# Attention scores in groups of 64 keys, q's decay from two small tables, and x's operands made in the order of use

## Chip, cores and metric

The kernel runs on one core of one Trainium2 chip. The metric is the device time of one execution in microseconds. Five engines work side by side on their own instruction streams: TensorE (PE; its weight loads are shown as PEld), VectorE (DVE), ScalarE (ACT), GpSimd (POOL) and SyncE (SP), which here issues nearly all DMAs. They meet at semaphores alone.

## The reference

Three stages follow each other. What the first computes is what the change mostly touches:

```python
gamma = 1.0 - 2.0 ** (-5.0 - np.arange(H, dtype=np.float32))
scale = 1.0 / np.sqrt(D)
state = np.zeros((B, H, D, D), dtype=np.float32)
for t in range(S):
    state = gamma[None, :, None, None] * state + np.einsum('bhd,bhe->bhde', k[:, :, t], v[:, :, t])
    y[:, :, t] = scale * np.einsum('bhd,bhde->bhe', q[:, :, t], state)
...
h = x @ w_in                                   # 3072 x 512 by 512 x 2048
g = np.where(h > 0.0, h, alpha * (np.exp(np.minimum(h, 0.0)) - 1.0))
x = g @ w_out                                  # back to 512
...
h = x @ w_in2                                  # 512 x 1024
solu = h * softmax(h); ln = layernorm(solu) * g_ln
out = ln @ w_out2
```

B = 4 sequences, H = 8 heads, S = 768 positions, D = 64. All inputs are float32.

## The kernel before

**Attention.** A sequence is cut into six chunks of C = 128 positions. A step s (there are NS = 12) takes the same chunk of two sequences. Inside a chunk the work is: `scores(s)`, K times Q for each of 8 heads and both sequences (16 matmuls of 64 rows, 128 keys by 128 queries); `key_values(s)`, the chunk's own K times V, for the state (16 matmuls, 128 rows by 64 by 64); `values(s)`, V times the masked scores A (16 matmuls); and `carried(s)`, the state from the chunk before times Q (16 matmuls of 64 by 64 by 128). Scores lie in PSUM with the key on the partition and the query on the free axis. DVE multiplies them by `causal`, a table of ones and zeros (`apply_mask`, line 877), so an entry whose query is before its key is computed and thrown away. Each float32 matmul appears in the trace as two weight loads and two matmul records, so that a group of 16 is "x32". PE goes through a step in the order scores, key_values, values, carried; in the first chunk of a pair of sequences (s = 0 and 6) there is no carried, and in the last (s = 5 and 11) it is scores, carried, values.

The decays are put into the operands: q is multiplied by gamma^(t+1)/8 (`decay_q`: DVE for s < EARLY = 2, POOL after that), v by its inverse (`decay_v`: ACT, and POOL for half of the heads at s < 2), and the state by gamma^128 (`decay_state`, POOL, line 492). q's table `q_decay` is 128 x 512. It is made on the chip: two rows `q_rows` are spread over 128 partitions by one float32 matmul (line 756) that stands between two series of warming matmuls on zeros (`WARM = (8, 4)`), DVE takes it from PSUM for step 0, and ACT copies it to SBUF for the others (line 1236).

**Loads.** Per step SP loads q, k, v and kn (k in its natural layout), 512 KB each, into one of three slots; step s + 3 is asked for when PE has ended step s (`load_step`, line 348). For s of 2 and more the order is q, v, k, kn. POOL's program in attention is, step by step: decay_q(s + 1), decay_state(s), at s = 6 and 7 two sums each for the first weights (`sum_u`), and from s = 9 on three `split_u_lo` each.

**The first MLP.** Both products are done to float32 precision from split operands (hi and lo parts, three matmuls for one), and the first by a Strassen-Winograd scheme with seven products M1 to M7 for each pair of features tiles n: `up_pair(n)`, which works in the order M1, M6, M2, M7, M5, M4, M3. Each product is six 128 x 128 x 512 matmuls (lines 656 to 658). Its right operands are seven tiles of x, called B11, B21, T1, T3, T2, B22, T4; their hi parts are made by ACT (line 1229) and their lo parts by DVE (`split_x_lo`, line 909) in the order of the list `MADE`. M1 needs B11, M6 needs T2, M2 needs B21, M7 needs T3, M5 needs T1, M4 needs T4, M3 needs B22. For the first block of 512 x-columns three lo parts are made inside the attention loop (s = 8, 9, 10) and four after it. `keep_u2(0)`, which adds M1 to M6 and on which M7 waits, stands on DVE behind these four.

Of the kernel before, what the change touches and what calls it, by code (L numbers as in the profile page):

```python
# [28 lines left out]
ND = 2 * NF1  # L29
WARM = (8, 4)  # L30
EARLY = 2
# [19 lines left out]

def build(nc, units, w1, w_in2, w_out2, g_ln, tables, q_table, x_dram, x2_dram, out):
    f32, f32r = mybir.dt.float32, mybir.dt.float32r
# [3 lines left out]
    with ctx:  # L57
# [72 lines left out]
        def two_chunks(name, at):  # L130
# [7 lines left out]
             for s in range(2)]  # L138
        decays = place("decays", C + 2 * H, f32, E_AT + 2 * K2)
        causal, v_decay, state_decay = decays[:, 0:C], decays[:, C:C + H], decays[:, C + H:C + 2 * H]  # L140

        y_at = [GH_AT, GH_AT + 4096, GH_AT + 8192, WLO_AT + 2 * K2, WLO_AT + 4 * K2, WLO_AT + 6 * K2,
# [5 lines left out]
        q_decay = place("q_decay", HH * C, f32, U3_AT)  # L148

        q_rows = place("q_rows", HH * C + P, f32, XL_AT)  # L150
        warm = place("warm", 512, mybir.dt.bfloat16, XH_AT)
# [15 lines left out]
        ps = ctx.enter_context(nc.psum_tensor("ps", [P, 8 * 512], f32))[:, :].rearrange("p (b c) -> p b c", c=512)  # L167

        def ps_scores(one, h):
            return ps[:, 2 * one + h // HH, (h % HH) * C:(h % HH + 1) * C]  # L170

# [46 lines left out]
        v_in = [sem(f"v_in{s}") for s in range(SLOTS)]  # L218
        q_rows_in = sem("q_rows_in")
        q_decay_spread = sem("q_decay_spread")  # L220
        q_decay_kept = sem("q_decay_kept")
        decays_in = sem("decays_in")
# [86 lines left out]

        MADE = [B11, B21, T1, T3, T2, B22, T4]  # L310
        SUMS = [T1, T3, T2, T4]
# [159 lines left out]
        def _(pool):  # L471
# [45 lines left out]
            for s in range(EARLY):  # L517
                decay_v(s)
            pool.wait_ge(q_decay_kept, 1)
            for s in range(NS):  # L520
# [59 lines left out]
        def _(pe):  # L580

            def scores(s):
                slot = s % SLOTS
                pe.wait_ge(k_in[slot], 16 * loads(s))
                for one in range(2):
                    if s < EARLY:
                        pe.wait_ge(q_early, 2 * s + one + 1)
                    else:
                        pe.wait_ge(q_decayed, 2 * (s - EARLY) + one + 1)
                    if s > 0:  # L590

                        pe.wait_ge(masked, 2 * s - 1 + one)
                    q, k = q_sb[slot][:, one, :], k_sb[slot][:, one, :]
                    for hh in range(HH):
                        for h in (hh, HH + hh):
                            c = slice(hh * C, hh * C + C)
                            last = nc.tensor.matmul(ps_scores(one, h), k[rows(h), c], q[rows(h), c], start=True, stop=True)  # L597
                    last.then_inc(scores_done, 1)
# [153 lines left out]
            pe.wait_ge(warm_zeroed, 1)  # L752
            for _ in range(WARM[0]):
                nc.tensor.matmul(ps[:, 6, :], warm[:, 0:P], warm[:, :], start=True, stop=True)
            pe.wait_ge(q_rows_in, 16)
            nc.tensor.matmul(ps[:, 7, :], q_rows[0:2, HH * C:HH * C + P], q_rows[0:2, 0:HH * C], start=True, stop=True)\
                .then_inc(q_decay_spread, 1)
            for _ in range(WARM[1]):
                nc.tensor.matmul(ps[:, 6, :], warm[:, 0:P], warm[:, :], start=True, stop=True)
            for s in range(NS):  # L760
# [107 lines left out]
        def _(dve):  # L868
# [44 lines left out]
            def decay_q(s):  # L913

                if s == 0:
                    dve.wait_ge(q_decay_spread, 1)
                else:
                    dve.wait_ge(q_decay_kept, 1)
                dve.wait_ge(q_in[s % SLOTS], 16 * loads(s))
                for one in range(2):  # L920
                    q = q_sb[s % SLOTS][:, one, :]
                    nc.vector.tensor_tensor(q, q, ps[:, 7, :] if s == 0 else q_decay[:, :], ALU.mult).then_inc(q_early, 1)

            decay_q(0)
            dve.wait_ge(decays_in, 16)
            for s in range(NS):
# [8 lines left out]
                elif 8 <= s < 11:  # L935
                    split_x_lo(0, s - 8)
            for i in range(3, 7):
                split_x_lo(0, i)

            def keep_sum(to, n, i, kept, bank, needs):  # L940
# [26 lines left out]
            def quadrants(n):  # L967
# [4 lines left out]
                h21 = p1[:, n % 2, :]  # L972
                if n != 1:
                    keep_u2(n)
# [30 lines left out]
            def w4_split_lo(f):  # L1005
# [3 lines left out]
                    .then_inc(w4_lo, 1)  # L1009

            for blk in range(NBLK):
                for i in range(NFP):
                    quadrants(NFP * blk + i)
                for f in range(1, NF1):
                    split_g_lo(down_no(blk, 1, f), stash[:, f, :])
                    if f == 3:
                        evacuate(blk, 0)
                    if 3 <= f < 7:
                        sum_x(blk + 1, f - 3)
                    if 7 <= f < 14:  # L1020
# [165 lines left out]
        def _(act):  # L1186
            act.dma_start(q_rows[0:2, :], q_table).then_inc(q_rows_in, 16)
            act.dma_start(decays[:, :], tables[:, T_DECAYS:T_DECAYS + C + 2 * H]).then_inc(decays_in, 16)

# [30 lines left out]
            def split_x_hi(blk, i):  # L1220
                o = MADE[i]
                if i == 0:
                    raw_ready(act, blk)
                if blk > 0 and o == B22:
# [8 lines left out]
            nc.scalar.activation(stats[0][:, 0:1], minus_half[:, :], ACT.Copy)  # L1233

            act.wait_ge(q_early, 2)
            nc.scalar.activation(q_decay[:, :], ps[:, 7, :], ACT.Copy).then_inc(q_decay_kept, 1)
            act.wait_ge(decays_in, 16)
# [186 lines left out]

T_DECAYS, T_IDENT = 0, C + 2 * H


def decay_tables():
# [5 lines left out]
    state_decay = np.tile(gamma[head] ** C, (1, 2))  # L1434
    parts = [causal, v_decay, state_decay, np.eye(P)]
    return np.concatenate(parts, axis=1).astype(np.float32)


def q_decay_rows():

    gamma = 1.0 - 2.0 ** (-5.0 - np.arange(H))
    decay = gamma[:, None] ** (np.arange(C) + 1.0)[None, :] / np.sqrt(D)
    half = np.arange(2)[:, None] == np.arange(P)[None, :] // D
    return np.concatenate([decay.reshape(2, HH * C), half.astype(np.float64)], axis=1).astype(np.float32)

# [34 lines left out]
```

## Time and profile before

| | |
|---|---|
| median of 3 runs | 839.67 us (839.61 to 840.21) |
| profiled execution: its time, its span | 839.78 us, 838.0 us |
| PE busy | 832.7 us, 99% of the span |
| DVE, ACT, POOL busy | 554.6, 415.5, 399.9 us |
| chain that ended last | PE 98%, DVE 1% |
| attention: first scores, last values | from 8.53 us to about 75.8 us |
| 16 DMA engines in the first four of 40 slices | 90% or more busy, 347 to 397 GB/s |
| the same in the other slices | mostly under 30% busy |

The span is divided by what limits it at each place. PE is busy nearly always, so time is won where PE has less to do or waits less. "Busy" of PE counts a matmul from its start to its modelled end, and matmuls overlap; the start of one group to the start of the next is the better measure of what a group costs. DMA is busy in the first tenth of the span alone, which is attention.

### The profile page before, as it was taken

The numbers are of one execution on the slowest core, as the hardware profiler recorded it, in microseconds if no ns is written. First come the engines' busy times: TensorE is split into PE (matmuls) and PEld (weight loads), VectorE is DVE, ScalarE is ACT, GpSimd is POOL, SyncE is SP. The second block draws the span as 40 slices with busy tenths as digits, with TensorE's granted clock in tenths as the row PEclk, the third lists the DMA queues.
The fourth block names the chain that finished last, engine by engine and source line by source line (L and its number), as shares of the span: only waits on it lengthen the run. The fifth ranks groups of instructions, "written<-read, shape, count | busy, mean of one in ns | idle before, by whom it ended". The sixth has DMA issues, their size and how long they took to land.

```text
span 838.0 us, 12616 instructions
## 1 busy us (share of the span) xinstructions
PE 832.7 (99%) x4854; PEld 691.8 (83%) x4854; DVE 554.6 (66%) x851; ACT 415.5 (50%) x671; POOL 399.9 (48%) x457
## 2 busy tenths in 40 slices
PE   9999999999999999999999999999999999999998
PEld 6998888888888888888888888888888888888886
DVE  4677767667635454575355555788977777777874
ACT  3685666665435655554455555563333343344322
POOL 3688766754026575620267651464334444444200
PEclk9999999999999999999999999999999999999999
DMA  9999211205002010140201001612111111111001
GB/s 347 392 397 353 97 57 51 75 26 179 1 15 87 26 51 25 36 166 1 75 26 51 27 26 50 201 51 75 51 51 51 51 50 39 51 51 51 13 25 51
DMA packets 49071, 73.31 MB, mean 87 GB/s; under 512 B 2930, under 2 KB 23666, under 8 KB 48756
## 3 DMA queue, kind: packets, MB, share of 16 engines
q1 hardware_dynamic: 48864, 72.43, 25.0%
q8 instruction: 39, 0.64, 0.3%
q14 instruction: 20, 0.16, 0.1%
q10 hardware_dynamic: 148, 0.08, 0.0%
HBM read 55.72 MB, written 16.78 MB: 87 GB/s over the span
## 4 chain that ended last, share of the span: by engine, by line
PE 98%; DVE 1%; issue 0%; ACT 0%; ACTq 0%
PE ps L703 10%; PE ps L707 10%; PE ps L704 10%; PE ps L656 9%; PE ps L658 9%; PE ps L657 9%; PE ps L827 5%; PE ps L825 5%; PE ps L826 5%; PE ps L715 5%; PE ps L717 5%; PE ps L716 5%; PE ps L597 3%; PE ps L811 3%; PE ps L625 2%; PE ps L612 1%
## 5 line engine op out<-in xcount | busy, mean ns | idle before, releaser
L513 POOL TENSOR_TENSOR u_lo<-u_raw,u_hi 128x256 fp32r<-128x256 f32 x168 | 142.0, 879 | 191.8 <-ACT u_hi L1218 191.8
L703 PE MATMUL ps<-g_hi,wd_hi 128*128 128x512 f32 x384 | 149.4, 389 | 0.0
L704 PE MATMUL ps<-g_hi,wd_lo 128*128 128x512 f32 x384 | 149.4, 389 | 0.0
L707 PE MATMUL ps<-g_lo,wd_hi 128*128 128x512 f32 x384 | 149.4, 389 | 0.0
L656 PE MATMUL ps<-x_hi,u_hi 128*128 128x512 f32 x336 | 131.5, 391 | 0.9 <-DVE u L942 0.9
L658 PE MATMUL ps<-x_lo,u_hi 128*128 128x512 f32 x336 | 130.8, 389 | 0.0
L657 PE MATMUL ps<-x_hi,u_lo 128*128 128x512 f32 x336 | 130.7, 389 | 0.0
L508 POOL TENSOR_TENSOR u_raw<-u_raw 128x256 f32<-128x256 f32 x96 | 90.8, 946 | 15.2 <-DMA u_raw<-w_dram 9.2
L554 POOL TENSOR_TENSOR u_lo<-x_raw,u_hi 128x256 fp32r<-128x256 f32 x84 | 66.0, 821 | 41.2 <-ACT u_hi L1340 41.2
L707 PEld LDWEIGHTS ps<-g_lo,wd_hi 128*128 128x128 f32 x384 | 72.1, 188 | 15.0
L704 PEld LDWEIGHTS ps<-g_hi,wd_lo 128*128 128x128 f32 x384 | 72.1, 188 | 15.0
L703 PEld LDWEIGHTS ps<-g_hi,wd_hi 128*128 128x128 f32 x384 | 72.1, 188 | 14.9
L656 PEld LDWEIGHTS ps<-x_hi,u_hi 128*128 128x128 f32 x336 | 63.0, 188 | 16.0 <-DVE u L942 1.6
L825 PE MATMUL ps<-wd_hi,n_hi 128*128 128x512 f32 x192 | 75.2, 392 | 0.0
L827 PE MATMUL ps<-wd_hi,n_lo 128*128 128x512 f32 x192 | 74.8, 389 | 0.0
L826 PE MATMUL ps<-wd_lo,n_hi 128*128 128x512 f32 x192 | 74.7, 389 | 0.0
L658 PEld LDWEIGHTS ps<-x_lo,u_hi 128*128 128x128 f32 x336 | 63.1, 188 | 13.2
L657 PEld LDWEIGHTS ps<-x_hi,u_lo 128*128 128x128 f32 x336 | 63.1, 188 | 12.9
L715 PE MATMUL ps<-x_hi,u_hi 128*128 128x512 f32 x168 | 66.5, 396 | 0.0
L717 PE MATMUL ps<-x_hi,u_lo 128*128 128x512 f32 x168 | 65.6, 390 | 0.0
L716 PE MATMUL ps<-x_lo,u_hi 128*128 128x512 f32 x168 | 65.4, 389 | 0.0
L1263 ACT ACTIVATE e<-e 128x512 f32<-128x512 f32 x96 | 60.7, 633 | 3.1
(94 smaller groups left out, 1447.8 us busy)
## 6 DMA issues: line engine op xcount, KB each, us to landing
u_raw<-w_dram SPq DMA_DIRECT2D x24, 512.0 KB, 3.5
q<-units_dram SPq DMA_DIRECT2D x12, 512.0 KB, 7.0
k<-units_dram SPq DMA_DIRECT2D x12, 512.0 KB, 8.5
v<-units_dram SPq DMA_DIRECT2D x12, 512.0 KB, 7.9
x_between<-x SPq DMA_DIRECT2D x24, 256.0 KB, 2.7
x_raw<-x_between SPq DMA_DIRECT2D x12, 512.0 KB, 3.6
out_dram<-y_sb SPq DMA_DIRECT2D x24, 256.0 KB, 2.0
kn<-units_dram SPq DMA_DIRECT2D x10, 512.0 KB, 9.7
```

What stands on the lines that cost most here:

```text
L513: nc.gpsimd.tensor_tensor(u_lo[n % 2][:, o, :], u_raw[n % 2][:, o, :], u_hi[n % 2][:, o, :].bitcast(f32), ALU.subtract).then_inc(ul_done, 1)
L656: nc.tensor.matmul(bank, hi, x_hi[:, b, k, :], start=(first and k == 0), stop=False, skip_group_check=True)
L657: nc.tensor.matmul(bank, lo, x_hi[:, b, k, :], start=False, stop=False, skip_group_check=True)
L658: done = nc.tensor.matmul(bank, hi, x_lo[:, b, k, :], start=False, stop=(k == 1), skip_group_check=True)
L703: nc.tensor.matmul(ps[:, bank + m, :], hi, g_hi[:, no % 3, :], start=(f == 0), stop=False)
L704: nc.tensor.matmul(ps[:, bank + m, :], lo, g_hi[:, no % 3, :], start=False, stop=False)
L707: last = nc.tensor.matmul(ps[:, bank + m, :], hi, g_lo[:, no % 3, :], start=False, stop=(f == NF1 - 1))
L715: nc.tensor.matmul(bank, x_h, hi, start=(first and k == 0), stop=False, skip_group_check=True)
L717: done = nc.tensor.matmul(bank, x_l, hi, start=False, stop=(k == 1), skip_group_check=True)
L825: nc.tensor.matmul(bank, n_hi[:, par, f, :], hi, start=(f == 0), stop=False)
L826: nc.tensor.matmul(bank, n_hi[:, par, f, :], lo, start=False, stop=False)
L827: last = nc.tensor.matmul(bank, n_lo[:, par, f, :], hi, start=False, stop=(f == NF2 - 1))
```

## The change

1. `scores`: each head's matmul of 128 keys by 128 queries is made two. Keys 0 to 63 are multiplied with all 128 queries, keys 64 to 127 with queries 64 to 127 alone. The corner that is left out (later keys, earlier queries) is multiplied by zero by the mask, as before; the warming matmuls now write zeros over banks 0 to 3, so it holds zeros or older finite scores.
2. q's decay: gamma^(t+1)/8 is the product of a table of 4 powers and one of 32 powers for each of 4 heads. Both come in the table `decays`, which grows from 144 to 288 columns, and DVE makes `q_decay` by one multiply. The input `q_rows`, its spreading matmul and ACT's copy are gone; 13 warming matmuls stand in one series.
3. `MADE` is B11, B21, T2, T3, T1, T4, B22, and `keep_u2(0)` moves ahead of the last `split_x_lo(0, 6)`. In later blocks the order of `MADE` alone changes.

```diff
-WARM = (8, 4)
+WARM = 13
+FINE = 32
+DECAYS = C + 2 * H + HH * (C // FINE + FINE)
...
-        MADE = [B11, B21, T1, T3, T2, B22, T4]
+        MADE = [B11, B21, T2, T3, T1, T4, B22]
...
                     for hh in range(HH):
-                        for h in (hh, HH + hh):
-                            c = slice(hh * C, hh * C + C)
-                            last = nc.tensor.matmul(ps_scores(one, h), k[rows(h), c], q[rows(h), c], start=True, stop=True)
+                        for late in range(2):
+                            for h in (hh, HH + hh):
+
+                                some = slice(hh * C + D * late, hh * C + D * late + D)
+                                rest = slice(hh * C + D * late, hh * C + C)
+                                last = nc.tensor.matmul(ps[D * late:D * late + D, 2 * one + h // HH, rest],
+                                                        k[rows(h), some], q[rows(h), rest], start=True, stop=True,
+                                                        skip_group_check=True)
                     last.then_inc(scores_done, 1)
...
-            for _ in range(WARM[0]):
-                nc.tensor.matmul(ps[:, 6, :], warm[:, 0:P], warm[:, :], start=True, stop=True)
-            pe.wait_ge(q_rows_in, 16)
-            nc.tensor.matmul(ps[:, 7, :], q_rows[0:2, HH * C:HH * C + P], q_rows[0:2, 0:HH * C], start=True, stop=True)\
-                .then_inc(q_decay_spread, 1)
-            for _ in range(WARM[1]):
-                nc.tensor.matmul(ps[:, 6, :], warm[:, 0:P], warm[:, :], start=True, stop=True)
+            for n in range(WARM):
+                nc.tensor.matmul(ps[:, n % 4, :], warm[:, 0:P], warm[:, :], start=True, stop=True)
...
+            dve.wait_ge(decays_in, 16)
+            parts = [P, HH, C // FINE, FINE]
+            nc.vector.tensor_tensor(q_decay[:, :].rearrange("p (h a b) -> p h a b", h=HH, b=FINE),
+                                    q_coarse.unsqueeze(3).to_broadcast(parts), q_fine.unsqueeze(2).to_broadcast(parts),
+                                    ALU.mult).then_inc(q_decay_made, 1)
+            dve.wait_ge(q_decay_made, 1)
             decay_q(0)
-            dve.wait_ge(decays_in, 16)
...
-            for i in range(3, 7):
-                split_x_lo(0, i)
-
...
-                if n != 1:
+                if n > 1:
                     keep_u2(n)
...
+            for i in range(3, 6):
+                split_x_lo(0, i)
+
+            keep_u2(0)
+            split_x_lo(0, 6)
             for blk in range(NBLK):
...
-            act.dma_start(q_rows[0:2, :], q_table).then_inc(q_rows_in, 16)
-            act.dma_start(decays[:, :], tables[:, T_DECAYS:T_DECAYS + C + 2 * H]).then_inc(decays_in, 16)
+            act.dma_start(decays[:, :], tables[:, T_DECAYS:T_DECAYS + DECAYS]).then_inc(decays_in, 16)
...
-            act.wait_ge(q_early, 2)
-            nc.scalar.activation(q_decay[:, :], ps[:, 7, :], ACT.Copy).then_inc(q_decay_kept, 1)
```

On PE, the beginning of the program before the change, from the warming matmuls over step 0 (names with a number are buffers of the three slots; the shape is that of the output):

```order
L754 MATMUL ps<-warm 128x512 x8
L756 MATMUL ps<-q_rows 128x512
L759 MATMUL ps<-warm 128x512 x4
L597 MATMUL ps<-q_79,k_82 128x128 x16
L612 MATMUL ps<-v_88,kn_85 64x64 x16
L625 MATMUL ps<-A_91,v_88 64x128 x16
```

And the same place after it, as far as the first of the eight repeats of the pattern go:

```order
L757 MATMUL ps<-warm 128x512 x13
L598 MATMUL ps<-q_79,k_82 64x128 x2
L598 MATMUL ps<-q_79,k_82 64x64 x2
L598 MATMUL ps<-q_79,k_82 64x128 x2
L598 MATMUL ps<-q_79,k_82 64x64 x2
L598 MATMUL ps<-q_79,k_82 64x128 x2
```

The 16 matmuls of a step's scores became 32, in eight pairs of pairs: two heads' early keys (in the two halves of the rows), then the same heads' late keys. The matmul on `q_rows` is gone, and one of the 13 warming matmuls takes its place.

On DVE, the end of attention and the start of the first MLP before the change (the lines from 942 on belong to up_pair(0); `u_75` is what keep_u2 writes, `u_76` what the next sum writes):

```order
L877 TENSOR_TENSOR A_92<-ps,decays 128x1024 [waits att_done,scores_done] x2
L909 TENSOR_TENSOR x_lo<-x_raw,x_hi 128x1024 [waits xh_done] x4
L942 TENSOR_TENSOR u_75<-p_74,ps 128x512 [waits part_done,p1_kept]
L942 TENSOR_TENSOR u_76<-p_74,ps 128x512 [waits part_done]
L947 SCALAR_TENSOR_TENSOR e<-e,ps 128x512 [waits e_done]
```

And after it:

```order
L875 TENSOR_TENSOR A_92<-ps,decays 128x1024 [waits att_done,scores_done] x2
L907 TENSOR_TENSOR x_lo<-x_raw,x_hi 128x1024 [waits xh_done] x3
L938 TENSOR_TENSOR u_75<-p_74,ps 128x512 [waits part_done,p1_kept]
L907 TENSOR_TENSOR x_lo<-x_raw,x_hi 128x1024 [waits xh_done]
L938 TENSOR_TENSOR u_76<-p_74,ps 128x512 [waits part_done]
L943 SCALAR_TENSOR_TENSOR e<-e,ps 128x512 [waits e_done]
```

Between the last mask and keep_u2 there are three splits in place of four. The rows don't tell it, but the first of them is now T3 (the tile for M7), and T2 (the tile for M6) is made inside the attention loop.

## Rows read from the trace of the kernel before

**Rows 1.** The page: chain of work that ended last, by engine.

```profile
PE 98%; DVE 1%; issue 0%; ACT 0%; ACTq 0%
```

**Rows 2.** Timeline of step 2, PE alone: start us, us, what, count.

```profile
19.98 2.06 PE L597 MATMUL ps<-q,k 64*128 64x128 f32 x32
...
21.96 1.15 PE L612 MATMUL ps<-v,kn 128*64 128x64 f32 x32
...
22.95 1.92 PE L625 MATMUL ps<-A,v 128*64 128x128 f32 x32
...
24.80 1.10 PE L642 MATMUL ps<-q,state 64*64 64x128 f32 x32
...
25.83 2.06 PE L597 MATMUL ps<-q,k 64*128 64x128 f32 x32
```

**Rows 3.** Groups by form, 20 to 70 us: count, busy us, mean ns.

```profile
L625 PE MATMUL ps<-A,v 128*64 128x128 f32 x288 | 17.3, 273 | 0.0
L612 PE MATMUL ps<-v,kn 128*64 128x64 f32 x256 | 9.2, 225 | 0.0
L642 PE MATMUL ps<-q,state 64*64 64x128 f32 x240 | 8.6, 276 | 0.0
```

**Rows 4.** Two stretches of 20 ns in L642: records in flight (x), clock, DMA.

```profile
24.92:24.94 0.02, 0.02 (x4) 1.00 1.08 410
24.98:25.00 0.02, 0.02 (x8) 1.00 0.53 205
```

**Rows 5.** Two stretches: busy us of PE, PEld, DVE, ACT, POOL; clock, DMA share, GB/s.

```profile
8.00:76.00 68.00, 68.00 (x1411) 62.24 (x1410) 47.02 (x46) 46.83 (x120) 52.30 (x44) 1.00 1.05 390
60.74:71.81 11.07, 11.07 (x250) 10.14 (x248) 8.51 (x8) 10.64 (x24) 11.07 (x10) 1.00 1.06 379
```

**Rows 6.** k's load for step 2: timeline, then issue to landing.

```profile
7.80 1.15 SPq L341 DMA_DIRECT2D k<-units_dram  x1
...
k<-units_dram SPq DMA_DIRECT2D x1, 512.0 KB, 11.8
```

**Rows 7.** k's load for step 9, its landing, and step 9's scores.

```profile
48.31 0.47 SPq L341 DMA_DIRECT2D k<-units_dram  x1
...
k<-units_dram SPq DMA_DIRECT2D x1, 512.0 KB, 9.8
...
58.96 0.38 PE L597 MATMUL ps<-q,k 64*128 64x128 f32 x2
```

**Rows 8.** q's load for step 10 and its landing; timeline of POOL and of PE's last carried.

```profile
53.24 0.37 SPq L341 DMA_DIRECT2D q<-units_dram  x1
...
q<-units_dram SPq DMA_DIRECT2D x1, 512.0 KB, 7.4
...
60.74 2.54 POOL L478 TENSOR_TENSOR q<-q,q_decay 128x512 f32<-128x512 f32 x2
...
69.79 2.02 POOL L492 TENSOR_TENSOR state<-state_sum,decays 128x512 f32<-128x512 f32 x1
...
72.84 1.10 PE L642 MATMUL ps<-q,state 64*64 64x128 f32 x32
```

**Rows 9.** Timeline of the first products; in brackets idle us before, and its releaser.

```profile
74.14 6.52 DVE L909 TENSOR_TENSOR x_lo<-x_raw,x_hi 128x1024 fp32r<-128x1024 f32 x4
...
75.77 0.19 PEld L656 LDWEIGHTS ps<-x_hi,u_hi 128*128 128x128 f32 x1 [0.17 <-issue]
...
77.43 0.19 PEld L656 LDWEIGHTS ps<-x_hi,u_hi 128*128 128x128 f32 x1 [0.43 <-issue]
...
78.00 0.19 PEld L656 LDWEIGHTS ps<-x_hi,u_hi 128*128 128x128 f32 x1
...
78.69 0.19 PEld L656 LDWEIGHTS ps<-x_hi,u_hi 128*128 128x128 f32 x1
...
81.32 0.19 PEld L656 LDWEIGHTS ps<-x_hi,u_hi 128*128 128x128 f32 x1 [1.27 <-DVE u L942]
```

**Rows 10.** Timeline: the matmul that spreads q's decay.

```profile
4.71 2.07 PE L756 MATMUL ps<-q_rows 2*128 2x512 f32 x2
```

More of the change, by code:

```diff
@@ L49, with build @@
 TILE_OF = {place_of(n): n for n in range(NCH)}
-def build(nc, units, w1, w_in2, w_out2, g_ln, tables, q_table, x_dram, x2_dram, out):
+def build(nc, units, w1, w_in2, w_out2, g_ln, tables, x_dram, x2_dram, out):
     f32, f32r = mybir.dt.float32, mybir.dt.float32r
@@ L138, in build @@
              for s in range(2)]
-        decays = place("decays", C + 2 * H, f32, E_AT + 2 * K2)
+        decays = place("decays", DECAYS, f32, E_AT + 2 * K2)
         causal, v_decay, state_decay = decays[:, 0:C], decays[:, C:C + H], decays[:, C + H:C + 2 * H]
+        q_coarse = decays[:, C + 2 * H:C + 2 * H + HH * (C // FINE)].rearrange("p (h a) -> p h a", h=HH)
+        q_fine = decays[:, C + 2 * H + HH * (C // FINE):DECAYS].rearrange("p (h b) -> p h b", h=HH)
         y_at = [GH_AT, GH_AT + 4096, GH_AT + 8192, WLO_AT + 2 * K2, WLO_AT + 4 * K2, WLO_AT + 6 * K2,
@@ L148, in build @@
         q_decay = place("q_decay", HH * C, f32, U3_AT)
-        q_rows = place("q_rows", HH * C + P, f32, XL_AT)
         warm = place("warm", 512, mybir.dt.bfloat16, XH_AT)
@@ L167, in build @@
         ps = ctx.enter_context(nc.psum_tensor("ps", [P, 8 * 512], f32))[:, :].rearrange("p (b c) -> p b c", c=512)
-        def ps_scores(one, h):
-            return ps[:, 2 * one + h // HH, (h % HH) * C:(h % HH + 1) * C]
         def ps_y(one, h):
@@ L218, in build @@
         v_in = [sem(f"v_in{s}") for s in range(SLOTS)]
-        q_rows_in = sem("q_rows_in")
-        q_decay_spread = sem("q_decay_spread")
-        q_decay_kept = sem("q_decay_kept")
+        q_decay_made = sem("q_decay_made")
         decays_in = sem("decays_in")
@@ L518, in _ @@
                 decay_v(s)
-            pool.wait_ge(q_decay_kept, 1)
+            pool.wait_ge(q_decay_made, 1)
             for s in range(NS):
@@ L913, in decay_q @@
             def decay_q(s):
[L915 to L918, printed above, removed]
                 dve.wait_ge(q_in[s % SLOTS], 16 * loads(s))
@@ L921, in decay_q @@
                     q = q_sb[s % SLOTS][:, one, :]
-                    nc.vector.tensor_tensor(q, q, ps[:, 7, :] if s == 0 else q_decay[:, :], ALU.mult).then_inc(q_early, 1)
+                    nc.vector.tensor_tensor(q, q, q_decay[:, :], ALU.mult).then_inc(q_early, 1)
+            dve.wait_ge(decays_in, 16)
[4 more added lines that the diff above has]
+            dve.wait_ge(q_decay_made, 1)
             decay_q(0)
-            dve.wait_ge(decays_in, 16)
             for s in range(NS):
@@ L1223, in split_x_hi @@
                     raw_ready(act, blk)
-                if blk > 0 and o == B22:
+                if blk > 0 and o == T4:
                     act.wait_ge(x2_stored[0], 16 * CB * blk)
@@ L1422, in _ @@
                 evacuate_y(t + 1)
-T_DECAYS, T_IDENT = 0, C + 2 * H
+T_DECAYS, T_IDENT = 0, DECAYS
 def decay_tables():
@@ L1434, in decay_tables @@
     state_decay = np.tile(gamma[head] ** C, (1, 2))
-    parts = [causal, v_decay, state_decay, np.eye(P)]
+    q_coarse = gamma[head][:, :, None] ** np.arange(0, C, FINE)[None, None, :]
+    q_fine = gamma[head][:, :, None] ** (np.arange(FINE) + 1.0)[None, None, :] / np.sqrt(D)
+    parts = [causal, v_decay, state_decay, q_coarse.reshape(P, -1), q_fine.reshape(P, -1), np.eye(P)]
     return np.concatenate(parts, axis=1).astype(np.float32)
[L1439 to L1444, printed above, removed]
 def kernel(q, k, v, moe_w_in, moe_w_out, moe2_w_in, moe2_w_out, moe2_g_ln):
@@ L1469 @@
         "tables": decay_tables(),
-        "q_table": q_decay_rows(),
     }
```

## The prediction, made before the changed kernel was run

> **What bounds the kernel now.** I read the page's chain first: 98% of what ended last is PE, 1% DVE [rows 1]. So a microsecond counts where PE has less to do or stops waiting, and the change touches PE at three places: the start, the scores in all twelve steps, and the first products after attention. Next the timeline of one step [rows 2]: scores start at 19.98, key_values at 21.96, values at 22.95, carried at 24.80, the next scores at 25.83. PE never stops; a step is 1.98 + 0.99 + 1.85 + 1.03 = 5.85 us. Then I asked what runs beside PE: from 8 to 76 us the DMA engines' share is 1.05 at 390 GB/s, and from 60.74 to 71.81 us POOL is busy 11.07 of 11.07 us [rows 5]. So attention has three resources close to full: PE, the load stream, and at its end POOL. The reader should see that a shorter PE step meets the other two. Last the transition [rows 9]: PE's first product begins at 75.77, the second at 77.43 after 0.43 us idle, and the fourth at 81.32 after 1.27 us idle with DVE as releaser.
>
> **Part 1, the scores.** The arithmetic falls by a quarter, but the array works in tiles, and the early-key tile decides. Values does 32 records on tiles of half the columns, two at a time: (1.92 - 0.27)/15 = 0.110 us from one pair to the next [rows 2, 3]. Carried does 32 records on four tiles of 64 by 64: four are in flight at 24.92 and eight at 24.98 [rows 4], so they start in waves of four, and (1.10 - 0.28)/7 = 0.117 us lies between waves, the slower first gap included [rows 2, 3]. A wave of 128 moving columns is 0.11 us whether it has two records or four. The new scores have 64 records. If two early and two late ones form a wave, there are 16 waves as long as the early records, 0.110 each: as many waves as before, no fewer. The quarter is saved in tiles that are not the longest. What does fall is the cost of changing shape. Old scores take 1.98 us from start to start, which is 15 x 0.110 = 1.65 plus 0.33 for getting in and out. New scores have the tile shape of carried, so where one follows the other nothing is emptied: about 1.85 for scores (0.13 less), and carried before them about 0.10 less than its 1.03. That is 0.23 for the 8 steps that follow a carried, about 0.1 for the other 4, and 0.15 more in each of the 2 steps where carried follows scores: 1.8 + 0.4 + 0.3 = 2.5 us if nothing else held PE. Bounds: at the low end of cost, the wave cannot be under carried's rate, so 2.5 us is about all there is; at the high end late records run after early ones, 16 waves at key_values' (1.15 - 0.225)/15 = 0.062 us [rows 2, 3] on top, 1.0 us per step. I take the overlap, because carried's form (same tiles, same two banks, two halves of the partitions) is the nearest row.
>
> The Trainium skill, in TensorEngine Tiling (Array Packing), Instruction Overhead, speaks against this: about 60 cycles of overhead per matmul, and no tiling factor to be had from a dimension that is small already. By it, an estimate: 32 more records a step at 60 cycles of 2.4 GHz, 25 ns each, is 0.8 us a step, 9.6 us in all, where I count a saving. By that rule the trace disagrees as far as it goes, since records of carried start four to a wave.
>
> **Part 2, where the scores' gain goes.** Loads are in one saturated stream, so their landings hardly move when PE asks sooner. k for step 2 is issued at 7.80 and lands 11.8 later, at 19.60 [rows 6], and scores of step 2 start at 19.98: PE can be at most 0.38 us earlier there. Part 3's start-up gain ends at this point. The larger table adds 144 columns x 128 x 4 bytes = 74 KB less 5 KB for q_rows, at 390 GB/s [rows 5] 0.18 us on every later landing; so 0.2 is left. From there a shorter step runs towards the stream: k for step 9 lands at 48.31 + 9.8 = 58.1 [rows 7], 58.3 with the table, and its scores start at 58.96: at most 0.7 earlier. The tightest is POOL. q for step 10 lands at 53.24 + 7.4 = 60.64, POOL starts on it at 60.74, has no idle moment until 71.81 [rows 5], when decay_state(10) ends (69.79 + 2.02), and the last carried needs that state; it starts at 72.84 [rows 8]. The change gives POOL neither less work nor an earlier q(10). With the table's 0.18, carried can't start before 72.0: 0.85 us earlier at most, and I take **0.8 us** for attention. Of the 2.5 + 0.2 the rest turns into waits of PE at the scores of steps 9 and 11 and at the last carried. To fill 0.8, the scores need to give only 0.06 us a step.
>
> **Part 3, the start.** The matmul on q_rows goes (2.07 us, [rows 10]), a warming one comes, DVE makes q_decay (not in the trace; between nothing, if k of step 0 lands later than it ends, and 1.27 us, POOL's 2.54 / 2 for such a multiply [rows 8]; it is a DVE operation, so nearer the middle: 0.7), and ACT's copy goes. PE may be one to two microseconds ahead in steps 0 and 1 and then waits for k of step 2, as above. Worth nothing of its own; it costs nothing either, unless it eats more than this lead.
>
> **Part 4, the transition.** The second product needs T2, now made inside the loop; the fourth needs T3 and keep_u2, which wait for three splits instead of four. Half a product is 78.69 - 78.00 = 0.69 us [rows 9], so three are 4.14 us and, with 0.1 for the first weights, the fourth could start 4.25 after the first; it starts 81.32 - 75.77 = 5.55 after. Gain **1.3 us**, if DVE is in time. It is: its splits are 6.52/4 = 1.63 each [rows 9]; they start at 74.14 now and about 0.8 to 1.0 earlier then (behind the last mask), so three end at 78.1 and keep_u2 at 78.8, while the fourth product comes up at 72.0 + (75.77 - 72.84) + 4.25 = 79.2. The slack is 0.4 us. The last split ends near 80.4, before M3 wants it at about 83.3. In later blocks the order of the list alone changes, and PE is the chain there; zero.
>
> **Sum.** 0.8 + 1.3 = 2.1 us of the profiled execution's 839.78 (span 838.0, 1.8 around it): 837.7. The median of the runs is 839.67, so the forecast is **837.6 us**. After the fourth product the kernel is PE's alone, so I expect the 2.1 us to arrive at the end undiminished.
>
> **Rivals.**
> - *The scores give nothing* (the extra records eat what the shape change saves): attention keeps only the 0.2 us of the start, the transition its 1.3: 838.2. Or DVE, with its slack of 0.4 us, is late for keep_u2 and the transition gives half: 838.3. For it: a wave has never mixed 128 and 64 moving columns in this trace. Against: only 0.06 us a step is needed.
> - *Late records don't run beside early ones* (the slower side). Place: each step's scores on PE. Price: 16 x 0.062 = 1.0 us a step, less the 0.2 of the shape changes, in twelve steps 9.6 us; less 1.3 of the transition and what was a wait anyway: about 847.5. It decides from 0.3 us a step on. The page named in part 1 would give the same sign. Against: rows 4's waves of four.
> - *The pins are looser than read*. If POOL's last chain (11.07 us, with multiplies slowed by DVE's work beside it) shortens, or landings come forward, the attention gain goes to 1.5 to 2.7: 835.7 to 836.9. For it: decay_state takes 2.02 us there, and its length may depend on what DVE does at that moment. Against: DVE has the same work to do in the same stretch.
> - *Warm-up or waits cost more*: PE now waits in steps 0 to 2. If the clock stayed low, or the new table came late, step 2 would still hide 1.5 us of it; a loss of more than that gives 838 to 840.
>
> **How the numbers follow.** A measurement of this kernel can tell about 0.2%, 1.7 us, from no change. Chances: the forecast (gain of 1.6 to 2.6) 0.60; scores or transition give less (gain 0.3 to 1.6) 0.22; looser pins 0.08; late records serial 0.07; dearer start 0.03. Faster by over 0.2% (under 838.0) is 0.56 of the first's 0.60, and the third's 0.08: 0.64. Slower is the serial case's 0.07 and 0.01 of the last: 0.08. The rest is within 0.2%: 0.28. The forecast's own range is 837.1 to 838.1. For eight in ten I take 836.4 to 839.1, which reaches into the looser pins and over the cases of a lesser gain, and leaves out the serial case.
>
> **What would show each step.** Scores of about 1.85 us start to start in step 3 and carried of about 0.93; the same total in PE's scores rows as waves of four. Waits of PE before the scores of step 2 (about 1 us), 9 and at the last carried, with POOL busy throughout the 11 us before. k of step 9 landing at 58.1 to 58.4. The fourth product 4.2 to 4.4 us after the first, without DVE as releaser. The forecast is wrong if scores take over 2.0 us, if POOL ends decay_state(10) before 71.4, or if keep_u2 still ends after 79.2.

## The result, and the profile after

The changed kernel takes 853.48 us (median of 4 runs, 851.28 to 854.87), the kernel before beside it 839.94 (4 runs, 839.61 to 840.25): 1.0156 times as long, 95% interval 1.0144 to 1.0168. It is slower by 13.5 us, far outside the forecast range. The profiled execution took 853.54 us, its span 851.7. From the page of the changed kernel, the slices, the instruction queue and the chain:

```profile
PE 829.9 (97%) x5237; PEld 690.4 (81%) x5237; DVE 559.2 (66%) x852; ACT 414.9 (49%) x670; POOL 397.5 (47%) x457
...
PE   8877999999999999999999999999999999999998
...
GB/s 345 351 333 302 192 50 100 50 37 132 58 1 75 50 25 48 28 155 19 0 99 25 50 26 1 222 75 55 57 62 40 48 49 50 50 50 43 20 25 50
...
q8 instruction: 42, 0.69, 0.3%
...
PE 95%; issue 2%; DMA 1%; DVE 1%; POOL 0%; SPq 0%; ACT 0%; DVEq 0%; ACTq 0%
```

PE is busy 2.8 us less than before (829.9 against 832.7) in a span 13.7 us longer. The loss lies in the first four slices, which is attention, and the chain has an entry that was 0% in [rows 1]: "issue", 2%, time in which PE waited for nothing that the profile shows. PE's first product of the MLP starts at 90.88 us, where [rows 9] has 75.77: 15.1 us are lost ahead of it and 1.4 are won behind it.

The timeline shows what a wait for "issue" looks like. Changed kernel, PE alone (start us, us, what, count, idle before):

```profile
19.73 1.48 PE L598 MATMUL ps<-q,k 64*64 64x128 f32 x45
22.40 0.66 PE L598 MATMUL ps<-q,k 64*64 64x64 f32 x19 [1.19 <-issue]
22.99 1.15 PE L615 MATMUL ps<-v,kn 128*64 128x64 f32 x32
23.97 1.92 PE L628 MATMUL ps<-A,v 128*64 128x128 f32 x32
25.82 1.10 PE L645 MATMUL ps<-q,state 64*64 64x128 f32 x32
26.75 0.60 PE L598 MATMUL ps<-q,k 64*64 64x128 f32 x11
28.43 1.58 PE L598 MATMUL ps<-q,k 64*64 64x128 f32 x53 [1.08 <-issue]
```

PE stops in the middle of a group, where the code has no wait: after 45 of 64 records of scores, then after 11 of 64, and next (34.56, past these rows) after 10 of 32 of carried. Between one stop and the next lie 19 + 32 + 32 + 32 + 11 = 126 matmul records and then 53 + 32 + 32 + 10 = 127. Counted in the trace with the weight loads and with the three or four semaphore instructions of PE's own that come between, each stop falls exactly 256 records after the last. Attention has eleven of them. At the weight loads, which stop first, they last 0.3 to 3.1 us, 18 us in all; at the matmuls, whose last ones are still running then, ten show and add up to 15.3 us. A window of 1 us on the DMA queues, 20.0 to 21.0 us, holds this:

```profile
q1 hardware_dynamic: 199, 0.38, 98.8%
q8 instruction: 1, 0.02, 6.0%
```

One packet of the instruction queue, 16384 bytes, which over 256 is 64 bytes for an instruction. It starts at 20.16, takes 0.95 us, and PE resumes at 22.40; the next start at 26.08 and 32.11, and PE resumes at 28.43 and 34.56. A resume comes 1.3 to 1.6 us behind the end of a packet. The other row, with 98.8%, is the kernel's own loads.

The Trainium skill, in Runtime: NRT & Kernel Launch, section Instruction fetch mechanics, describes a queue of this kind: instructions are refilled in blocks of 16 KiB, 256 instructions, by a DMA queue of the sequencer's own, and crossing a block is "mostly hidden". The block size agrees with the packet of 16384 bytes and the 256 records between stops. "Mostly hidden" does not hold here, with 18 us of stops.

The list of PE's waits in the changed kernel up to 90 us (us in total, times, longest) has the same 15.3 us under "issue"; waits for data come to 2.0 us for v and, at the weight loads, 0.5 for k:

```profile
PE ps L598 <- issue: 5.7, 4, 2.3
PE ps L615 <- issue: 3.7, 3, 2.2
PE ps L645 <- issue: 3.1, 2, 1.9
PE ps L628 <- issue: 2.8, 1, 2.8
```

Where no stop falls, the step is what the prediction said. Steps 10 and 11, PE alone:

```profile
79.73 1.10 PE L645 MATMUL ps<-q,state 64*64 64x128 f32 x32
80.66 1.92 PE L598 MATMUL ps<-q,k 64*64 64x128 f32 x64
82.50 1.15 PE L615 MATMUL ps<-v,kn 128*64 128x64 f32 x32
83.49 1.92 PE L628 MATMUL ps<-A,v 128*64 128x128 f32 x32
85.34 1.10 PE L645 MATMUL ps<-q,state 64*64 64x128 f32 x32
86.26 1.81 PE L598 MATMUL ps<-q,k 64*64 64x128 f32 x62
```

Carried to scores 0.93, scores 1.84, key_values 0.99, values 1.85: against [rows 2] 0.24 us less a step. The 64 records of scores go through in the time of 16 waves of 0.115 us (four records side by side).

The transition, changed kernel, start us, us, what:

```profile
89.65 5.00 DVE L907 TENSOR_TENSOR x_lo<-x_raw,x_hi 128x1024 fp32r<-128x1024 f32 x3
90.88 0.19 PEld L659 LDWEIGHTS ps<-x_hi,u_hi 128*128 128x128 f32 x1 [0.17 <-issue]
...
94.57 0.68 DVE L938 TENSOR_TENSOR u<-p,ps 128x512 f32<-128x512 f32 x1
...
95.30 0.19 PEld L659 LDWEIGHTS ps<-x_hi,u_hi 128*128 128x128 f32 x1 [0.47 <-DVE u L938]
```

The fourth product starts 4.42 us after the first, where [rows 9] has 5.55 and the prediction 4.25.

### The profile page after: what moved, and what is told of

It reads as the page before. It is cut to its first block, busy times and chain, and to the rows that moved or that the text cites. A ratio compares the mean times of both kernels' runs of the same rounds, so it can differ in the third digit from the quotient of the medians.

```text
span 851.7 us, 13382 instructions
## 1 busy us (share of the span) xinstructions
PE 829.9 (97%) x5237; PEld 690.4 (81%) x5237; DVE 559.2 (66%) x852; ACT 414.9 (49%) x670; POOL 397.5 (47%) x457
## 4 chain that ended last, share of the span: by engine, by line
PE 95%; issue 2%; DMA 1%; DVE 1%; POOL 0%; SPq 0%; ACT 0%; DVEq 0%; ACTq 0%
PE ps L707 10%; PE ps L710 10%; PE ps L706 10%; PE ps L659 9%; PE ps L661 9%; PE ps L660 9%; PE ps L823 5%; PE ps L824 5%; PE ps L825 5%; PE ps L718 5%; PE ps L720 4%; PE ps L719 4%; PE ps L809 2%; PE ps L598 2%; PE ps L628 2%
## 5 line engine op out<-in xcount | busy, mean ns | idle before, releaser
L506 POOL TENSOR_TENSOR u_raw<-u_raw 128x256 f32<-128x256 f32 x96 | 88.5, 922 | 14.4 <-DMA u_raw<-w_dram 8.4
```

## The experiments

**Theory F** (fetch): PE's instructions come in blocks of 256, and while the load stream keeps the DMA engines full PE gets a block only every 6 to 7 us. The step before needs 256 instructions in 5.85 us (64 matmuls, each two weight loads and two matmuls). The changed step has 80 matmuls, 320 instructions, for which PE would take 5.61 us. PE's few semaphore instructions come on top in both. **The rivals**: the new scores' records themselves are dear on the array or on PE's sequencer (theory S for their shape, theory A for the array's time alone); the new start or the new order breaks something (rival G); PE waits for data, which the trace puts down to "issue". Each run was timed beside the kernel before on its chip, whose medians were 839.59 to 840.17.

**Which part is it?** e1_scores_alone is the kernel before with part 1 of the change only (the eight first warming matmuls go to banks 0 to 3). e2_without_scores is the changed kernel with the old scores. e3_order_alone is the kernel before with the new list and place of keep_u2.

```diff
e1: -  c = slice(hh * C, hh * C + C)
    +  for late in range(2): ... 64 keys by 128 or by 64 queries
e2: the same lines the other way round, in the changed kernel
e3: -        MADE = [B11, B21, T1, T3, T2, B22, T4]
    +        MADE = [B11, B21, T2, T3, T1, T4, B22]
```

> The kernel before with part 1 alone (scores in groups of 64 keys; the first eight warming matmuls write zeros to banks 0 to 3 so that the corner left out is finite). Theory F (instruction fetch): PE's instructions arrive in blocks of 16 KB, 256 instructions, and in attention such a block takes 6 to 7.7 us because the DMA engines are full; scores in pieces make a step 320 PE instructions instead of 256, so PE stops at each block's end. It expects nearly the whole loss here: 10 to 14 us slower than before, 850 to 854 us, and stops of 1 to 3 us exactly 256 PE instructions apart. Rival G (the start): PE, being ahead at the start, runs into loads and blocks that are late; it expects 838 to 841 us, as the start is the old one. Rival S (shape): the mixed waves themselves stall PE; it expects the loss here too, but stops at places of scores, not every 256 instructions.

> The changed kernel with the old scores (16 matmuls of 128 keys by 128 queries): parts 2 and 3 of the change alone. Theory F: a step has 256 PE instructions again and the blocks keep up, or nearly: 837.5 to 839.5 us, no or few stops 256 instructions apart; PE being ahead at the start might make one or two stops show. Rival G expects the loss of 10 us or more here. Rival S expects 837.5 to 838.5.

> The kernel before with the order of operands alone (MADE and the place of keep_u2). The prediction's part 4 says 1.3 us less: 838.4 to 838.7 us, the fourth product 4.2 to 4.4 us after the first. The changed kernel's own trace has 4.42 with 0.47 of it a wait for DVE, so 1.1 to 1.3 less is expected by every theory; if the time stays at 839.7, the wait is only moved behind the fourth product.

Measured: e1 855.69 us, ratio 1.0185 (1.017 to 1.020). e2 837.83, 0.9973 (0.9962 to 0.9983). e3 839.25, 0.9989 (0.998 to 0.9998). So the scores alone are the loss, and all else together gains 2.2 us. e2 is inside F's range; e1 is 1.7 us above its 854, and e3 gains 0.8 us where 1.0 to 1.3 had been expected. The timeline of e1 has PE's longest stop in it, again inside a group:

```profile
56.64 0.27 PE L617 MATMUL ps<-v,kn 128*64 128x64 f32 x1
60.58 1.09 PE L617 MATMUL ps<-v,kn 128*64 128x64 f32 x30 [3.67 <-issue]
```

That group is key_values, which the change does not touch: the stop goes with the count of instructions and not with the new form. e2 and e3 have one small stop each, within step 11's scores. With PE's records (matmuls, weight loads, semaphore instructions) numbered from the start of the program, it falls on the same one, number 2754, as the changed kernel's stop at 71.7 us and one stop each of e1, e4, e8 and e11, though the instruction at that place differs. e2's (0.24 us of idle) stands in its timeline, and so does the fourth product's start, 4.02 us after the first at 75.37 and without a wait:

```profile
71.92 0.60 PE L595 MATMUL ps<-q,k 64*128 64x128 f32 x5 [0.24 <-issue]
...
79.39 0.19 PEld L654 LDWEIGHTS ps<-x_hi,u_hi 128*128 128x128 f32 x1
```

**Is it the load stream?** From step 3 on, e4_light_loads brings only 64 of the 512 columns of v and kn, e5_before_light_loads does so in the kernel before, and e10_hardly_any_loads brings 64 of 512 of all four in the changed kernel. The rest of each tile keeps older values; all instructions of PE stay as they were.

```diff
-  to[s % SLOTS], units[n:n + NC + 1:NC, :, 512 * i:512 * (i + 1)]
+  w = 64 if s >= SLOTS and i >= 2 else 512      # e10: w = 64 if s >= SLOTS else 512
+  to[s % SLOTS][:, :, 0:w], units[n:n + NC + 1:NC, :, 512 * i:512 * i + w]
```

> The changed kernel, in which v's and kn's loads bring 64 of 512 columns for steps 3 and later (the rest of these slots is old data, so the output is not the reference's); all instructions and waits are the same, and the DMA engines have some 45% less to carry in attention. Theory F: a block of instructions comes sooner than PE needs it, the stops go, and the scores' gain and the start's come out: 833 to 837 us. Rival S: the stops stay where they are, 850 us or more. Rival G: as F.

> The kernel before with the same light loads (v and kn bring 64 of 512 columns for steps 3 and later; the output is not the reference's). It is the base for the changed kernel with light loads. Since PE hardly waits in attention before, every theory expects 839 to 840 us, at most some 0.4 us less; the difference of the two with light loads is then what the change is worth without the full DMA engines: by the prediction's terms 2.5 for scores, 1.3 for the order and 1 to 2 for the start, together 4 to 5.5 us.

> The changed kernel with all four loads of the steps from 3 on brought down to 64 of 512 columns (the rest of the slots is old data; the output is not the reference's). With v and kn alone so, a block still took 5.3 to 5.9 us and 846.6 us came out, where 833 to 837 had been expected. If the time of a block is waiting behind data, it falls under 4.5 us here and no stop is left: 833 to 837 us. If it is mostly a fixed latency of the fetch, blocks stay at 5 us or more and the time at 842 to 846.

Measured: e4 846.59 us, 1.0082 (1.0065 to 1.0099). e5 839.56, 0.9993 (0.9984 to 1.0002). e10 838.36, 0.998 (0.9971 to 0.999). e4 missed what was expected: fewer bytes made the stops shorter but left them, and against e5 the change still costs 7.0 us. The stretch from 36 to 60 us shows it (busy us of PE and PEld with their records in brackets, DVE, ACT, POOL; clock, DMA share, GB/s). The kernel before:

```profile
36.00:60.00 24.00, 24.00 (x510) 21.97 (x506) 16.83 (x16) 18.51 (x47) 20.03 (x16) 1.00 1.04 389
```

The changed kernel:

```profile
36.00:60.00 24.00, 18.69 (x497) 16.78 (x493) 14.44 (x14) 16.91 (x44) 12.76 (x10) 1.00 0.94 332
```

e4_light_loads:

```profile
36.00:60.00 24.00, 21.98 (x590) 19.97 (x587) 17.01 (x17) 18.03 (x46) 18.66 (x15) 1.00 0.78 244
```

e10_hardly_any_loads:

```profile
36.00:60.00 24.00, 23.90 (x684) 22.11 (x681) 18.67 (x18) 19.05 (x47) 21.37 (x16) 1.00 0.31 72
```

Add the two counts in brackets, x of PE and of PEld: 1016, 990, 1177 and 1365 PE instructions in 24 us, so 256 of them in 6.0, 6.2, 5.2 and 4.5 us. In e10 that is PE's own pace (5.61 x 256/320 = 4.5), and its steps run without a stop. Its timeline, one step:

```profile
26.32 1.92 PE L599 MATMUL ps<-q,k 64*64 64x128 f32 x64
...
31.01 1.10 PE L646 MATMUL ps<-q,state 64*64 64x128 f32 x32
31.93 1.92 PE L599 MATMUL ps<-q,k 64*64 64x128 f32 x64
```

The same PE instructions that cost 13.5 us over the kernel before cost nothing over it once the loads are nearly gone. Rivals of dear records fall with this pair. e10 did not reach the 833 to 837 expected. Two stops of 0.6 and 1.2 us at the weight loads come up to 22 us, while full loads are still under way, and one of 2.2 up to 69.05, when the MLP's loads fill the queues (1.10 of the engines, 340 GB/s from 64 to 66.7 us); behind it the clock is low (last section).

**Is it the number of instructions?** Four runs change that number or what stands between instructions. In e9_half_pieces only one of the two sequences has the new scores: 288 instructions a step. e8_query_halves is the kernel before with each scores matmul cut into two of 64 queries: 320, with the old arithmetic. e11_small_matmuls is the kernel before with 16 extra small matmuls a step: 320. e6_extra_waits has, behind key_values, 64 waits on a semaphore long satisfied, in ten steps.

```diff
e9:  +  if one == 0: (the new loops)  else: (the old loop)
e8:  +  for part in range(2): ... k[rows(h), c], q[rows(h), some]        # 128 keys by 64 queries
e11: +  few = slice(hh * C, hh * C + 8)
     +  nc.tensor.matmul(ps[0:D, 2 * one + h // HH, few], k[rows(h), hh * C:hh * C + D], q[rows(h), few], ...)
e6:  +  for _ in range(64):
     +      pe.wait_ge(consts_set, 1)
```

> The changed kernel with pieces for the first of the two sequences alone and whole scores for the second: 288 PE instructions a step, between 256 (837.8 us without pieces) and 320 (853.5). In the changed kernel ten blocks took 63.0 us, 6.3 each. With about 3250 instead of 3650 instructions up to the first MLP, theory F expects its start near 84 to 85 us, for 75.4 and 90.9: 843 to 849 us. Theory S expects half of the loss too, with another two changes of shape a step; the places of the stops tell the two apart, every 256 instructions or at scores.

> The kernel before with its own score shape (128 keys, 64 rows), but each matmul cut into two of 64 queries: 32 matmuls, so 64 more PE instructions a step, as in the changed kernel, without its tiles of 64 by 64 and without mixed waves. In waves of 0.058 us for 64 columns it costs the array 32 x 0.058 = 1.87 us a step for 1.79, 1 us in all. Theory F (instruction fetch) expects stops every 256 PE instructions again and 852 to 856 us. Theory S (shape) expects 840.5 to 842 us without such stops.

> The kernel before, whose scores send behind their 16 matmuls another 16 of 64 keys by 8 queries, which write 8 columns a second time with the same values. A step has then 320 PE instructions, as in the changed kernel, with nearly no more columns to move, the old decay and the old loads. The extra 32 records in carried's tile shape cost the array at most carried's 1.03 us a step, and with 8 columns in place of 128 rather 0.5. Theory F (PE's instructions come in blocks of 256, and beside full DMA engines a block takes 6 to 7.7 us): the steps of attention last as long as in the changed kernel, 852 to 858 us, with PE stopping within a group at every 256th record of PE and PEld together. Theory A (the array's time alone counts): 12 x 0.3 to 0.7 us more, 843.5 to 848.5, and no stops inside a group.

> The kernel before with 64 more PE instructions per step that do no array work: waits on a semaphore that is long satisfied, behind key_values in the 10 steps that have it. Theory F: a step has 320 PE instructions as in the changed kernel, so PE stops at the ends of blocks in attention: 8 to 14 us slower, stops 256 instructions apart, anywhere in a step. Rival S: array and shape are unchanged, so at most what the sequencer needs for 64 waits, if the queue doesn't hide it (a bubble at the same place of each step): 0 to 6 us.

e9: 850.01 us, 1.0119 (1.0085 to 1.0152), 1.0 us above F's range of 843 to 849: half the extra instructions, nearly three quarters of the loss. From 28 us on it has seven stops, all at multiples of 256 records from one another.

e8: 866.61, 1.0294 (1.0223 to 1.0365), above every expectation. Its timeline says why:

```profile
20.14 3.79 PE L599 MATMUL ps<-q,k 64*128 64x64 f32 x64
23.86 1.15 PE L615 MATMUL ps<-v,kn 128*64 128x64 f32 x32
...
27.73 3.79 PE L599 MATMUL ps<-q,k 64*128 64x64 f32 x64
```

64 records of half as many columns take 3.72 us where 32 of full width take 1.98 [rows 2]: halving the queries halves nothing. Twelve times 1.74 is 20.9 of the 26.4 us. A step is 7.59 us, so 256 instructions take 6.1, about what the supply gives, and PE hardly stops: 2.1 us at record 2754 and 0.5 at 3266. As a test of F the run decides nothing, since both F and the array's time can give it. Its four runs lie between 857.63 and 870.36, and nothing here says why.

e11: 858.34, 1.0236 (1.0201 to 1.0271). Its timeline:

```profile
29.14 0.60 PE L597 MATMUL ps<-q,k 64*128 64x128 f32 x6 [0.61 <-issue]
29.67 0.64 PE L601 MATMUL ps<-q,k 64*64 64x8 f32 x16
30.24 1.16 PE L597 MATMUL ps<-q,k 64*128 64x128 f32 x16
31.33 0.64 PE L601 MATMUL ps<-q,k 64*64 64x8 f32 x16
31.89 1.15 PE L617 MATMUL ps<-v,kn 128*64 128x64 f32 x32
32.87 1.92 PE L630 MATMUL ps<-A,v 128*64 128x128 f32 x32
34.72 0.54 PE L647 MATMUL ps<-q,state 64*64 64x128 f32 x9
36.16 0.88 PE L647 MATMUL ps<-q,state 64*64 64x128 f32 x23 [0.90 <-issue]
```

Here the old scores, the old start and the old order have the same stops: 6 + 16 + 16 + 16 + 32 + 32 + 9 = 127 matmul records from stop to stop, and six such stops of 0.4 to 1.4 us at the weight loads (5.3 us in all), which the kernel before does not have. F expected the stops and theory A none, so A falls as the whole account. In size F missed: 16 records of 8 columns take 0.57 us and not the 0.25 assumed, so the array adds about 1.3 us a step, some 16 of the 18.8 us, and the sum is a little above F's range. That the stops are shorter than after the change fits a step of 7.2 us, which asks for less.

e6: 883.95, 1.0513 (1.0491 to 1.0535). Its timeline (PEld) shows the waits as "issue" of another kind, at one place in the step and never inside a group:

```profile
25.80 2.78 PEld L627 LDWEIGHTS ps<-A,v 128*64 128x64 f32 x32 [2.94 <-issue]
```

The run is far above what either theory expected, and its edit did half of what was meant: the page counts 12936 instructions against 12616 before, 320 more for the 640 waits in the code. PE idles 2.8 to 3.0 us before values in each of the ten steps, some 29 us, and the rest of the 44 us is mostly the clock: in nine of the ten the granted clock fell to 0.50 behind the idle time, and values took 3.15 us here and 3.52 a step later, instead of 1.92. The step became 10.5 us long, so its instructions came in time. The run tells nothing for or against F; it shows that "issue" can also be the sequencer's own work.

**Can the loads be held back?** e7_throttle2 and e7_throttle3 are the changed kernel with at most two or three loads under way.

```diff
+  if len(issued) >= 2:
+      sp.wait_ge(*issued[-2])
```

> The changed kernel, with loads of attention issued only when the load but one before has landed, so at most two (1 MB) are under way in place of four or more. Theory F: a block of instructions waits behind less data, so it comes faster than the 6 to 7.7 us; if the data stream is not starved by it, the stops shrink and the time is 838 to 848. If two under way are too few to fill the engines (each load now needs 7 to 10 us from issue, of which 1.27 is its own), loads come late and steps wait for k: over 850.

> The same with at most three loads (1.5 MB) under way. Theory F: between the changed kernel and the one with two: stops shorter than 1.3 to 3 us, 842 to 851, with less danger of starving the loads. If the fetch of a block does not depend on how much data is queued ahead of it, both stay at 851 to 855.

Measured: 878.13 us, 1.0458 (1.0442 to 1.0474), and 857.93, 1.0212 (1.0183 to 1.0242). Both are slower than the changed kernel: e7_throttle2 is the case "over 850" that had been named for late loads, and e7_throttle3 is above both of its ranges. With two loads under way the waits of e7_throttle2 from 8 to 92 us are:

```profile
PEld ps L604 <- DMA k<-units_dram: 19.7, 8, 4.0
...
PEld ps L621 <- issue: 2.1, 7, 0.5
```

The long waits for issue are nearly gone, as F has it, but k comes late by up to 4.0 us a time, and the granted clock drops too (0.86 from 36 to 60 us). With three loads under way there are both: 11.4 us of waits for k at the weight loads, and stops of up to 2.0 us on the 256-record places. Holding the loads back gains nothing here.

## Why the prediction was wrong

**The step that failed** is part 1's sum, "2.5 us if nothing else held PE", together with its high bound. It priced the new scores by the array's waves alone. A matmul more is also four instructions more to bring in, and the term is missing on every side: in the sum, among the bounds, among the rivals. It measures, in the changed kernel, 18 us of stops less the 3 us or so that scores and start gave: 15.1 us at the first product. That the kernel before ran 256 instructions per 5.85 us, without a stop, while its DMA share was 1.05 [rows 5], could be read from its trace, and so could how little was to spare. From 19 to 72 us each packet of its queue "instruction" ends only 1.3 to 2.9 us before PE comes to the record that begins the next 256; 1.3 is the shortest time from a packet's end to a resume in the changed kernel. Nobody asked what that queue carries.

**Part 1's mechanism** was right. Scores take 1.84 us from start to start with 64 records (1.86 in e10), carried 0.93 before them: forecast 1.85 and 0.93. The rival of late records behind early ones (847.5 us) came nearest to the time by its sign and is wrong as a mechanism: 16 waves are all there are. The rule of the Trainium skill that stood beside it (TensorEngine Tiling (Array Packing), Instruction Overhead) had the sign too, by an estimate of 0.8 us a step on the array; where nothing stops PE the step is 0.24 us shorter than before, in the changed kernel and in e10.

**Part 2's pins** never came to bear in the changed kernel: from its stops on, PE was later than k, q(10) and POOL. POOL, which had no idle moment from 60.74 to 71.81, is busy 10.27 of the 16 us from 60 to 76. In e2, where scores are the old ones, the first product starts at 75.37, 0.4 us earlier than before, and two of the pins prove looser than read. Step 2's scores wait 0.94 us for k (forecast about 1), but start at 19.09, 0.89 us earlier than before, where at most 0.38 was allowed. POOL ends decay_state(10) at 70.82, not at 71.81, though the forecast said that the change gives POOL no earlier q(10):

```profile
68.79 2.03 POOL L490 TENSOR_TENSOR state<-state_sum,decays 128x512 f32<-128x512 f32 x1
```

Whether 0.8 would have been reached with the new scores is open, since no run had both them and full loads without stops.

**Part 3, the start**, was worth little, as forecast: q_decay takes DVE 0.69 us (forecast 0.7), and the first scores begin at 6.54 instead of 8.53, which the waits for v in steps 0 and 1 and the first stop nearly take back (step 2's scores start at 19.73, for 19.98).

**Part 4, the transition**, was right in its gain and wrong in its slack. After the first product the changed kernel needs 760.8 us to the end of the span, the kernel before 762.2: 1.4 us won, forecast 1.3. In the changed kernel the fourth product waits 0.47 us for keep_u2, since DVE's first split starts 1.23 us before the first product (1.63 in [rows 9]) and its three splits take 1.67 us each rather than 1.63. The later start goes with the new scores and not with the stops: step 11's scores to the first product is 4.62 us on PE (86.26 to 90.88) where it was 5.11, and DVE's masks in between take as long as before. e10 has the same 1.22 us between first split and first product; its three splits take 4.09 us together, and nothing waits. In e2 they start 1.68 us before, nothing waits, and the fourth product comes 4.02 us after the first. So the prediction moved DVE's start with PE's and missed that shorter scores leave DVE less time; "PE's alone" held behind it.

**The best of all runs** is e2, the change without its scores: 837.83 us, 0.9973 of the kernel before. It probably owes most of it to the order of the operands, 1.5 us by the fourth product (4.02 after the first, for 5.55). e3 has that alone and loses 0.5 us of it again to one stop of the block kind in step 11:

```profile
72.63 0.71 PE L597 MATMUL ps<-q,k 64*128 64x128 f32 x6 [0.54 <-issue]
```

**Shown and argued.** Shown: stops come every 256 PE instructions, with the packets of the instruction queue. In the changed kernel, e1 to e4 and e8 to e11, every stop of attention that lasts over 0.3 us at the matmuls under the name "issue" falls on record 194 of PE's stream or a multiple of 256 behind it, give or take one, whatever stands there. Stops appear with more instructions a step (changed kernel, e1, e9, e11) and shrink with the bytes loaded beside them (e4, e10). Shown too: the time that goes is that between PE's passing a 256-record place and the start of the next packet, since the packet itself takes 0.9 us. In the changed kernel this is 3.7 to 5.2 us up to 77 us, in e10 0.4 to 1.2 us between 22 and 58. It is 1.8 us once in the changed kernel's own stream, from 34.56 on, where the loads had nearly run dry, and 1.0 to 1.5 us after 79 us, behind the last loads of attention, although the engines are full there (stretches as above):

```profile
34.50:36.30 1.80, 1.74 (x68) 1.75 (x70) 0.00 (x0) 0.81 (x2) 1.22 (x1) 1.00 0.22 91
79.40:80.80 1.40, 1.40 (x44) 1.23 (x48) 0.00 (x0) 0.00 (x0) 1.40 (x2) 1.00 1.13 343
```

So the share of the DMA engines alone doesn't set it. Argued only: what does. A place behind the descriptors of the kernel's large loads would do it; no run looks inside the queues.

## What to carry to other kernels

Where small float32 matmuls run beside a saturated load stream, count PE's instructions (four for each matmul) per microsecond as well as its columns. Here PE kept up with 256 in 5.85 us and not with 256 in 4.5. Stops inside a group, labelled "issue" and equally far apart in records, are the sign; fewer instructions, or fewer bytes at that time, are the cure, and cutting a matmul in two to save columns is the opposite. A piece of a float32 matmul with half the columns may also cost as much as the whole, so measure a wave before halving it.

## What the runs showed of the hardware

- **Instruction supply of PE.** Blocks of 16384 bytes on a queue of their own, one for 256 instructions, about 0.9 us each, and PE goes on 1.3 to 1.6 us behind its end. PE got a block in 6.2 us beside 332 GB/s of loads, in 5.2 beside 244, and in 4.5, its own pace, beside 72. GB/s alone do not tell it: in the same stretch it was 6.3 us in e1 beside 297, and 6.7 in e9 beside 356.
- **Fewer columns don't always shorten a small record.** A pair with 128 keys as weights takes 0.116 us with 64 queries (e8, 3.72/32) and 0.124 with 128 (1.98/16, [rows 2]); a record of 64 keys by 8 queries takes 0.036 us (0.57/16, e11), one by 128 queries in carried 0.032 (1.03/32, [rows 2]). It is not so for every shape: key_values' pair has 0.062 us with 64 columns, values' 0.110 with 128 [rows 3]. No run tells what sets it.
- **A satisfied wait on PE** isn't free: 64 of them in the code, half as many in the trace, left PE idle for 2.8 to 3.0 us, some 45 ns for each in the code (e6).
- **A long stop can cost the clock too.** After 3.7 us without a matmul in e1 and 2.1 in e10 the granted clock fell to the lower of its two levels (0.50, 1.2 GHz), and e1's values took 3.40 us instead of 1.92. Stretches of e1 as above:

```profile
60.50:63.00 2.50, 2.42 (x48) 2.42 (x49) 1.24 (x2) 0.00 (x0) 0.47 (x1) 0.76 1.06 410
63.00:65.00 2.00, 2.00 (x23) 1.67 (x23) 0.59 (x1) 0.00 (x0) 2.00 (x2) 0.50 0.75 288
```

In the changed kernel the clock stayed at 1.00 behind its longest stop, 2.8 us without a matmul, and in e6 it fell behind nine of ten idle stretches of 2.8 to 3.0 us. The length of a stop alone doesn't tell what the clock does.
